# Sorting the MLP's rows by expert, scattering expert results by row, and splitting the first MLP weights inside the expert loop

## What is computed

```
x = attention(q, k, v)              # 4 batches x 8 heads x 576 tokens x 64, causal, window of 64
skip = x @ w_skip                   # a token is computed only if skip > 0, else it passes unchanged
e = argmax(x @ w_gate)              # one of 8 experts per token, gate = softmax at e
x[t] += gate[t] * (relu(x[t] @ w1[e]) @ w2[e])        # w1 512x1024, w2 1024x512, for computed tokens
h = x @ w_in                        # 512x2048
out = (h * clip(h + 3, 0, 6) / 6) @ w_out             # 2048x512, every row on its own
```

## Time and profile before

| | |
|---|---|
| median of 3 runs | 686.51 us (684.18 to 686.89) |
| profiled execution | 687.68 us, span of its instructions 686.1 us |
| PE busy | 645.8 us (94%), mean granted clock 0.982 |
| DVE, ACT, POOL busy | 396.7 (58%), 323.6 (47%), 71.7 us (10%) |
| DMA | 95.10 MB, 139 GB/s over the span |
| stages | attention to about 122 us, expert loop 132 to 280 us, MLP from 292 us |

### The profile page before, as it was taken

How to read it: one execution, slowest core, us unless ns; L and a number is a source line. 1 busy time by engine, 2 the same in 40 slices (tenths; PEclk the granted TensorE clock), 3 DMA queues, 4 the chain that set the end, 5 groups by cost and what they waited for, 6 DMA issues and landing times.

```text
span 686.1 us, 17259 instructions
## 1 busy us (share of the span) xinstructions
PE 645.8 (94%) x6528; PEld 559.3 (82%) x6528; DVE 396.7 (58%) x1043; ACT 323.6 (47%) x675; POOL 71.7 (10%) x122
## 2 busy tenths in 40 slices
PE   5899996779999999889999999999999999999998
PEld 4788874757777887778988989888988988888986
DVE  2677875201111111568777768877777688777753
ACT  3799874011111111474554455644555566454433
POOL 4333452311111111000000000000000000000000
PEclk9999997889999999999999999999999999999999
DMA  9788869688577158632222221533222214222102
GB/s 161 170 192 198 202 189 393 204 296 302 182 275 275 31 202 272 203 114 63 76 77 78 61 64 60 200 107 94 92 62 63 61 60 156 63 61 63 32 0 93
DMA packets 118818, 95.10 MB, mean 139 GB/s; under 512 B 62737, under 2 KB 94485, under 8 KB 118752
## 3 DMA queue, kind: packets, MB, share of 16 engines
q1 hardware_dynamic: 103280, 61.79, 31.9%
q10 hardware_dynamic: 12496, 26.11, 11.1%
q0 software_dynamic: 2976, 6.32, 2.7%
HBM read 80.01 MB, written 17.52 MB: 142 GB/s over the span
## 4 chain that ended last, share of the span: by engine, by line
PE 80%; DMA 7%; DVE 6%; issue 3%; ACT 1%; SPq 1%; another core or an unknown queue 1%; POOL 0%; POOLq 0%; DVEq 0%; ACTq 0%
PE bank L1007 29%; PE av L956 25%; PE av L932 8%; PE bank L920 8%; DMA xin<-x_rows 5%; PE av L777 3%; DVE sm L1360 2%; PE bank L733 2%; PE bank L793 2%; PE bank L718 1%; PE av L889 1%; DVE xall L1373 1%; DMA ot<-x_new 1%; PE av L944 1%; DMA qraw<-in_q 1%
## 5 line engine op out<-in xcount | busy, mean ns | idle before, releaser
L1007 PE MATMUL bank<-o_hi,g_lo 128*128 128x512 f32 x288 | 114.7, 398 | 0.0
L1007 PE MATMUL bank<-o_lo,g_hi 128*128 128x512 f32 x288 | 114.2, 397 | 0.0
L1007 PE MATMUL bank<-o_hi,g_hi 128*128 128x512 f32 x288 | 112.5, 391 | 0.0
L956 PE MATMUL av<-xc_hi,w_hi 128*128 128x384 f32 x342 | 89.3, 342 | 2.2 <-issue 1.9
L956 PE MATMUL av<-xc_hi,w_lo 128*128 128x384 f32 x342 | 87.7, 337 | 0.0
L956 PE MATMUL av<-xc_lo,w_hi 128*128 128x384 f32 x342 | 87.4, 336 | 0.0
L956 PEld LDWEIGHTS av<-xc_hi,w_hi 128*128 128x128 f32 x342 | 62.5, 189 | 18.1 <-issue 2.7
L1622 DVE TENSOR_TENSOR g_lo<-act,g_hi 128x384 fp32r<-128x384 f32 x96 | 53.4, 556 | 40.2 <-ACT g_hi L1234 37.1
L920 PEld LDWEIGHTS bank<-xeT,w1s 128*64 128x64 f32 x2176 | 68.6, 138 | 6.9 <-issue 4.6
L1234 ACT CAST g_hi<-act 128x384 fp32r<-128x384 f32 x96 | 49.4, 515 | 50.9 <-DVE act L1615 50.9
L920 PE MATMUL bank<-xeT,w1s 128*64 128x64 f32 x2176 | 70.9, 223 | 2.1 <-issue 1.0
(11 more groups left out here) (157 smaller groups left out, 914.7 us busy)
## 6 DMA issues: line engine op xcount, KB each, us to landing
w2s<-in_moe_w ACTq DMA_DIRECT2D x7, 2048.0 KB
wor<-in_moe_w_out SPq DMA_DIRECT2D x24, 512.0 KB, 3.6
w1s<-in_moe_w ACTq DMA_DIRECT2D x5, 2048.0 KB, 16.0
wir<-in_moe_w_in SPq DMA_DIRECT2D x24, 256.0 KB, 4.2
wir<-in_moe_w_in SPq DMA_DIRECT2D x48, 128.0 KB, 4.0
qraw<-in_q SPq DMA_DIRECT2D x36, 128.0 KB
vnow<-in_v SPq DMA_DIRECT2D x36, 128.0 KB
x_new<-xall SPq DMA_DIRECT2D x18, 256.0 KB
```

Source lines behind the costliest of these rows:

```text
L956: last = pe.matmul(into[:, 0:GN], a[it % 2][:, W_AT[w], c, :], b[:, X_AT[x], c, :], start=(n == 0 and fresh), stop=(n == 3 * XQ * len(pair ...
L1007: last = pe.matmul(bank[tile][:, :], a[c][:, i * P:(i + 1) * P], b[it % 2][:, units(it)[c], :], start=(plain(it) and c in (0, 2) and n == ...
```

## The change

The tensor `x_new` is gone, and with it its 18 stores. `x_rows` gets N rows in front (R0 = N + ET), which the MLP reads. A ninth column (NC = NE + 1) in the one-hot `oh` counts the skipped tokens. Of the first twelve tiles (NTS), skipped tokens are scattered straight to the first rows, followed by room for each expert's tokens; `shift` moves an expert's row to its place there. The last six tiles (one MLP group) keep their token order. All 2304 rows are scattered now. Expert results (`yo`, now with its 4 extra columns) are scattered to the row `yrow`. The MLP's results of the first twelve tiles are scattered by POOL to the token that stands in each row (`tok`), from six buffers `ot`; the last six are stored as before.

SP waits ahead of the first x tile only for the experts whose first sorted row is below 768 (`needed`). Routing worked out from the reference's inputs gives 881 skipped tokens in the first twelve tiles, so `needed` is 0 here. The loads and splits of the weights of MLP iterations 0 and 1 go into the expert loop, at its experts 4 to 7, except `w_low(1)`, which goes into iteration 0. The `idle_turns` behind the loop are gone.

```diff
@@ SP, from the attention's end to the MLP
-            sp.wait_ge(s_xst, 16 * NT)
-            sp.wait_ge(s_yst, total * 16 + YS0)
+            sp.wait_ge(s_yst, before_first * 16 + YS0)
             for i in range(MT):
                 load_x(0, i)
...
+                if it == 0:
+                    sp.wait_ge(s_yst, total * 16 + YS0)
...
                 if e == 0:
                     sp.wait_ge(s_scat, 16 * NT)
-                    sp.wait_ge(s_pad0, 16)
+                    sp.wait_ge(s_pad0, 16 * 2)
+                elif e == 4:
+                    sp.wait_ge(s_padp, 16 * (NE - 5))
+                    sp.wait_ge(s_yst, YS0)
+                    load_w_in(0)
+                elif e == 5:
+                    load_w_out(0)
+                elif e == 6:
+                    load_w_in(1)
+                elif e == 7:
+                    load_w_out(1)
@@ PE
-            idle_turns(4)
-            total = tile_bound(pe, NE)
-            pe.wait_ge(s_xetc, total + 1)
-            fixed(pe)
-            idle_turns(3)
             for i in range(MT):
                 transpose_tile(0, i)
+            pe.wait_ge(s_xetc, end + 1)
+            pe.wait_ge(s_yc, end + YC0)
+            fixed(pe)
@@ ACT
-            padding(sc, range(0, 1), s_pad0)
-            padding(sc, range(1, 4), s_pad)
+            pads = pad_rows(sc, range(4))
+            padding(sc, pads[:2], s_pad0)
...
             sc.wait_ge(s_xet, 1 + XT0)
             take_xe()
+            padding(sc, pads[2:], s_pad)
             load_w2(sc, 1, s_wp2[1])
...
+                if e == 4:
+                    w_high(0)
+                    w_rest_high(0)
+                elif e == 5:
+                    o_high(0)
+                elif e == 6:
+                    w_high(1)
+                elif e == 7:
+                    w_rest_high(1)
@@ DVE, expert loop
-                    dve.tensor_copy(ytok[:, :], xres[:, TOKEN:TOKEN + 1])
+                    dve.tensor_copy(yo[:, DH:HW], xres[:, DH:HW])
+                    dve.scalar_tensor_tensor(out=yrow[:, :], in0=xres[:, FLAG:FLAG + 1], scalar=shift[:, e:e + 1],
+                                             in1=xres[:, ROW:ROW + 1], op0=ALU.mult, op1=ALU.add)
...
+                if e == 4:
+                    w_low(0)
+                elif e == 5:
+                    o_low(0)
+                elif e == 6:
+                    combine_w(1)
@@ DVE, MLP iteration 0
                     activate(0, 0)
                     first_low(4)
                     first_low(5)
+                    w_low(1)
                     low(0, 0)
@@ POOL, MLP
+            for T in range(NTS):
+                take_tokens(T // MT, T % MT)
+            for T in range(NTS):
+                pool.wait_ge(s_tok, T + 1)
+                pool.wait_ge(s_oca, T + 1)
+                pool.indirect_dma_start(out=out, out_offset=bass.IndirectOffsetOnAxis(ap=tok[:, T:T + 1], axis=0),
+                                        in_=ot[T % MT][:, :], in_offset=None, bounds_check=N - 1, oob_is_err=False).then_inc(s_ost[T % MT], 16)
```

More of the change, by code:

```diff
@@ L119, in attention_moe_mlp_kernel @@
         at["X"] = 0
-        xn = [put("X", f"xn{i}", [P, DM]) for i in range(3)]
+        xn = [put("X", f"xn{i}", [P, 2, HW]) for i in range(3)]
         g_hi = [put("X", f"g_hi{i}", [P, GN], fp32r) for i in range(4)]
@@ L553, in load_w_out @@
                 sp.dma_start(wor[it % 2][:, :, :], halves[:, :, it % FP, :]).then_inc(s_wor[it % 2], 16)
+            sp.wait_ge(s_tbl, 1)
+            for e, first, end in expert_tiles(sp, first_bounds(sp)):
+                if e == 0:
+                    sp.wait_ge(s_scat, 16 * NT)
+                    sp.wait_ge(s_pad0, 16 * 2)
+                elif e == 2:
+                    sp.wait_ge(s_pad, 16 * 2)
+                elif e == 4:
[8 more added lines that the diff above has]
+                    load_w_out(1)
+                with sp.Fori(0, end - first) as t:
+                    g = first + t
+                    row = t * ET + (R0 + e * R)
+                    sp.wait_ge(s_xet, g + XT0)
+                    sp.wait_ge(s_xmid, g + XM0)
+                    load_rows(bass.ds(row, ET))
+            total = end
+            sp.wait_ge(s_first, 1)
+            before_first = sp.value_load(needed[0:1, 0:1], min_val=0, max_val=TMAX)
+            sp.wait_ge(s_xet, total + XT0)
+            sp.wait_ge(s_xmid, total + XM0)
+            load_rows(slice(R0, R0 + ET))
             def load_x(G, i):
@@ L1178, in o_high @@
                         wor[it % 2][:, :, :].rearrange("p u n -> p (u n)")).then_inc(s_ohi, 1)
+            sc.wait_ge(s_xet, 1 + XT0)
+            take_xe()
+            padding(sc, pads[2:], s_pad)
+            load_w2(sc, 1, s_wp2[1])
+            for e, first, end in expert_tiles(sc, bounds):
+                with sc.Fori(0, end - first) as t:
+                    g = first + t
+                    for m in range(FC // 2):
+                        sc.wait_ge(s_h, g * (FC // 2) + m + 1)
+                        sc.activation(hT[:, 2 * m:2 * m + 2, :], bank[m % 4][:, 0:2 * ET].rearrange("p (f s) -> p f s", f=2),
+                                      ACT.Relu).then_inc(s_hc, 1)
+                    sc.wait_ge(s_xet, g + 2 + XT0)
+                    take_xe()
+                if e == 4:
[7 more added lines that the diff above has]
+                    w_rest_high(1)
+                if e + 2 < NE:
+                    sc.wait_ge(s_y, end)
+                    fixed(sc)
+                    if e == 0:
+                        sc.wait_ge(s_scat, 16 * NT)
+                    load_w2(sc, e + 2, s_wp2[(e + 2) % 3])
+                if e + 3 < NE:
+                    load_w1(sc, e + 3, s_wp1[e % 3])
             def take_x(G, i):
```

319 lines of the change are left out of this document (151 added, 168 removed).

## The result

The changed kernel takes 681.88 us (median of 20 runs, 677.51 to 684.70); the kernel before took 685.62 us beside it (20 runs, 681.52 to 688.70). The ratio is 0.9944, 95% interval 0.9924 to 0.9963: about 3.8 us (2.5 to 5.2) faster where 10.5 were forecast. A second timing on another chip gave 0.9924 (0.9897 to 0.9952). The profiled executions are 681.86 us now against 687.68 before.

What follows compares the result with a forecast made beforehand. The prediction took PE as the bound for the most part, with two holes left, the first expert tile and the hand-over. Its terms -6.4 - 4.9 + 0.8 = -10.5 us gave 676.0 us, range 671.5 to 682.5 us.

Steps and rivals of the forecast that it cites:

- term 2: First expert tile: pads issued ahead of w2 let the second `xin` land in time; -4.9 us, bounds -6.4 and -3.3.
- Term 1: Hand-over from expert loop to MLP: early x loads close the hole from 12.5 to 4.3 us; -6.4 us with `w_low(1)`.
- the group has 2.0 us for three tiles, six are 4.0 us: Hand-over: PE's transposes of six x tiles sized from a group of three; 4.3 us with issue.
- `w_low(1)`: MLP iteration 0: its 2.2 us on DVE, hidden in the hole before, delay iteration 1; 1.8 us lost.
- I give back two of them, 1.5 us: Expert loop: later `xin` waits of PE, 3.1 us for four, about 0.8 each; two of them lost again.
- Winning the second `xin`: First expert tile: 4.5 us of PE's waiting and 1.9 us of slow clock won, together 6.4 us.
- Term 3: Start of the expert loop: larger last scatter, one more DVE operation and a wait for two pads; +0.8 us, bounds +0.2 and +2.5.
- the second pad: Start of the loop: SP now waits for it, and it lands 0.2 us behind the last scatter.
- the last scatter: Start of the loop: carrying all 128 rows of a tile, it takes 0.4 us more.
- The late `xin`, 680.9 us: Rival, first expert tile: order of issue does not hold the second `xin`, PE's wait and slow product stay; chance 0.20.
- the sum at -5.6 us: Under the skill's queue rule, issue order moves nothing and the first-tile gain is 0; ground of the first rival, chance 0.20.
- Slower by `yo`'s landing: Rival, expert loop: `yo` scattered into 1040-byte rows lands later, each of 17 tiles costs; d = 6 gives 703 us; chance 0.05.

Runs made afterwards that it cites:

- e8: Changed kernel, but the first loads of the MLP's rows wait for every expert result, as in the kernel before; 1.0051 of the kernel before.
- e2: Changed kernel with ACT issuing the load of expert 1's w2 ahead of pads 2 and 3; 0.9928 of the kernel before.
- e3: Changed kernel with the kernel before's order of pads, expert 1's w2 load right behind the copy of xeT; 0.9941 of the kernel before.
- e7: Changed kernel with POOL waiting for three tiles' rows instead of two before loading w1 of expert 2; 1.0014 of the kernel before.
- e6: Changed kernel with the three `xn` tiles placed behind `g_hi`, `g_lo`, `p1`, `usum` and `hq`; 0.9901 of the kernel before.
- e12: Kernel before with a 96-byte gap behind its three `xn` tiles, nothing else; 1.0020 of the kernel before.
- e4: Changed kernel with `w_low(1)` moved from iteration 0 into the expert loop, its load issued at expert 5; 0.9876 of the kernel before.
- e10: The program of e4 run once more for a second trace; not timed, MLP 392.00 us.
- e11: Changed kernel with two repairs, `w_low(1)` in the expert loop and `g_hi` at an even place; 0.9885 of the kernel before.
- e9: Changed kernel with expert 2's w1 load moved from POOL to ACT, right behind expert 1's w2; 0.9900 of the kernel before.

## Why the prediction was wrong

The direction was right, and the time lies within the range. The gain of 3.8 us is less than half of the forecast, and what failed is term 2. The traces fall 4.3 us short of the forecast: 3.6 in term 2, 1.5 by the address of `g_hi`, 1.0 ahead of the first tile, less 1.7 that the hand-over won beyond its forecast. The rest of the gap to the medians lies in how far the traced executions of the kernel before stood above its medians.

- **Term 1, the hand-over: right, and undersized.** The hole closed by 9.7 us, not 8.2. The step "the group has 2.0 us for three tiles, six are 4.0 us" failed: there each tile waited for its load and stood alone; back to back, at the same granted clock of 1.00, the six tiles took 2.84 us. `w_low(1)` cost 1.57 us against 1.8. Term 1 as forecast was -6.4, measured -8.1; e8 takes it back.
- **Term 2, the first expert tile: the step that failed** is "I give back two of them, 1.5 us". Winning the second `xin` was right (no wait, product at 3.67 us; e2 and e3 bring it back). What came later was priced from other tiles' waits for `xin` alone, and these were misread: of the 7.6 us, 1.75 are the wait for the first `xin`, ahead of the first tile, so the later ones sum to 1.4 us, not 3.1, and are 0.86, 0.36 and 0.15, none of them in the third tile. In its place the runs show four prices: the third `xin` (a wait of 1.3 to 2.3 us in the seven traces), w2 of expert 1, which lands 14.8 to 15.4 us after its issue where it delays the tile (0 to 2.1 us), a second product behind these waits that in three of the seven traces takes 5.2 to 6.5 us instead of 3.67 (granted clock 0.72 in the changed kernel), and a first product of 5.2 to 5.5 us instead of 3.95 in five of them.

  The third `xin` and w2 are late together. POOL issues its 2 MB, w1 of expert 2, when two `xin` have landed, so a second `xin` that is early starts this load early: at 138.35 us instead of 142.55, beside w2 of expert 1, and it took 15.85 us to land instead of 10.17 (e2, where the second `xin` is late again: 143.16 and 10.57). e7 moves it away, and the third tile waits for no weights.

  For the term as a whole the table has -3.7 + 2.4 = -1.3 us against -4.9, and e3 shows that even this is not the order's doing. So the forecast's 4.9 us for the order were 0 within what the traces can tell. What makes the stretch 2.1 us shorter than before in the mean (two traces against seven that spread over 3.2 us), with either order, stays open.
- **Term 3, the start: +1.2 us against +0.8, within its bounds.** SP did wait for the second pad: it was sent at 126.64 us and landed at 129.8, 0.3 us behind the scatter, as forecast (0.2). What was sized too low is the last scatter: it carries all 128 rows of its tile now and takes 0.8 us longer to land, not 0.4, in the mean of two traces each. The pad, which e3 takes away, is worth 0.2 to 0.3 us. That the rows alone make the scatter slower was not tried. Ahead of the ranking product another 0.6 us appear in the means, within the spread of the traces.
- **Missing: the address, +1.3 to +1.9 us.** The forecast has no term for the wider `xn` tiles and did not ask what they move behind them.
- **The rivals.** The late `xin`, 680.9 us, came closest in time, but not as a mechanism: the second `xin` was early and the others paid. By the rule of the Trainium skill that the engines go round between queues (DMA: Bandwidth & Descriptors, section Queues, rings and completion order), the prediction had term 2 at 0 and the sum at -5.6 us. That sum is near the -6.2 us of the traces, the reason right only in part: e2 and e3 show that the order of two issues moves a wait of 2.6 to 3.8 us to another tile, yet not the total. Slower by `yo`'s landing did not happen: DVE's wait for it went from 61.3 us to 67.7 in 16 times, and PE did not wait for it, except in e7.

The profiled execution of before was 2.1 us above its later median of 685.62 us, of which the forecast had taken off 1.2.

## What to carry to other kernels

A stall at the start of a stretch whose transfers are all due is worth only what the last of them gives back: before a small transfer is moved ahead, list the large ones behind it, with what their engine and their queue hold, and those that its landing sets off. Where a change widens one tile, check where the tiles behind it begin, above all those that PE reads in the longest loop. And take two traces of the same program before a difference of 2 us is given a cause.

## What was not expected of the hardware

- Output products whose weights (`g_hi`, `g_lo`) begin 96 bytes further on take 1.40 us for six instead of 1.39, at the granted clock of 1.00; in both kernels (e6, e12). `g_hi` and `g_lo` were not moved apart from each other.
- Waiting often costs twice. In the third tile 1.91 us of idle time (e4: 1.52 + 0.39) left the second product at 3.67 us, with 2.90 us (changed kernel) it took 5.24, with 3.94 us (e10) 6.53. The length alone does not decide: 2.29 us (e6) left 3.67, 2.16 us (e11) went with 5.36. The granted clock of the changed kernel from 150 to 156 us is 0.72, between the levels of 1.2 and 2.4 GHz.
- A DMA issue by ACT can block it for 6.52 us (e9) after three loads of 2 MB issued by it within 7.7 us, and for 4.47 us after two (e10); SP's third 2 MB load took 5.84 us to issue in the changed kernel. What is queued behind such an issue on its engine waits too.
